# Order at the seams of token blocks in a fused attention and two-MLP kernel: low part ahead of the gate, weight split behind it, sum banks released singly

## The reference

```python
for t in range(S):
    y[:, :, t] = einsum('bhd,bhde->bhe', r[t], state + outer(u * k[t], v[t]))
    state = w[t][..., None] * state + outer(k[t], v[t])
h = x @ moe_w_in                      # first MLP, x from y
x = (h * clip(h + 3, 0, 6) / 6) @ moe_w_out
h = x @ moe2_w_in                     # second MLP
out = (h * sigmoid(h)) @ moe2_w_out
```

## Time and profile before

| | |
|---|---|
| time, median of 3 runs | 937.94 us (937.28 to 940.25) |
| the profiled execution | 939.23 us |
| its span, first to last instruction | 937.5 us |
| mean granted TensorE clock | 0.978 |
| PE busy | 905.1 us, 97% |
| DVE, ACT, POOL busy | 467.1, 320.2, 155.7 us |
| first seam of a step / stage seam | about 141 us / about 534 us |

### The profile page before, as it was taken

One profiled execution on the slowest core, in us unless ns is written; L12 is line 12 of the kernel. 1 busy time (PEld: TensorE's weight loads), 2 busy tenths in 40 slices (PEclk: granted clock), 3 DMA queues, 4 the chain that ended last, 5 costly groups with the idle time before them and its releaser, 6 DMA issues.

```text
span 937.5 us, 15408 instructions
## 1 busy us (share of the span) xinstructions
PE 905.1 (97%) x5876; PEld 776.2 (83%) x5876; DVE 467.1 (50%) x692; ACT 320.2 (34%) x537; POOL 155.7 (17%) x154
## 2 busy tenths in 40 slices
PE   5479999999999999999999999999999999999998
PEld 4468888887888888788888799998999989999897
DVE  5866746664674666467445542342333333333332
ACT  1343323333333333333344632333332332332332
POOL 6553413231341333134000000000000000000000
PEclk7679999999999999999999999999999999999999
DMA  8561221113123111311202200000000000000000
GB/s 250 174 184 38 74 76 45 55 55 99 46 63 82 37 55 55 99 59 51 100 7 96 68 1 1 35 0 0 34 0 0 34 0 0 34 0 0 34 1 34
DMA packets 13367, 48.54 MB, mean 52 GB/s; under 512 B 1568, under 2 KB 2208, under 8 KB 13344
## 3 DMA queue, kind: packets, MB, share of 16 engines
q1 hardware_dynamic: 13344, 48.23, 16.6%
HBM read 43.50 MB, written 4.72 MB: 51 GB/s over the span
## 4 chain that ended last, share of the span: by engine, by line
PE 92%; DVE 2%; DMA 2%; issue 1%; POOL 1%; ACT 1%; SPq 0%; POOLq 0%; ACTq 0%
PE bank L679 14%; PE bank L680 14%; PE bank L681 14%; PE bank L691 7%; PE bank L703 7%; PE bank L705 7%; PE bank L704 7%; PE bank L692 7%; PE bank L693 7%; PE bank L739 2%; PE bank L770 2%; PE bank L775 1%; DMA x<-u_row 1%; PE bank L752 1%; PE bank L727 1%
## 5 line engine op out<-in xcount | busy, mean ns | idle before, releaser
L679 PE MATMUL bank<-x_hi,w_hi 128*128 (+1 forms) x576 | 227.6, 395 | 1.7 <-DVE x_lo L590 1.7
L680 PE MATMUL bank<-x_lo,w_hi 128*128 (+1 forms) x576 | 227.0, 394 | 0.0
L681 PE MATMUL bank<-x_hi,w_lo 128*128 (+1 forms) x576 | 226.9, 394 | 0.0
L397 ACT CAST g_hi<-g 128x512 fp32r<-128x512 f32 x192 | 119.2, 621 | 284.2 <-PE bank L705 144.2
L517 DVE TENSOR_TENSOR g<-g,bank 128x512 f32<-128x512 f32 x96 | 65.9, 687 | 244.4 <-ACT g L391 244.4
L524 DVE TENSOR_TENSOR g_lo<-g,g_hi 128x512 fp32r<-128x512 f32 x192 | 147.7, 769 | 0.9 <-ACT g_hi L397 0.9
L703 PE MATMUL bank<-w_hi,g_hi 128*128 128x384 f32 x384 | 129.5, 337 | 0.0
L705 PE MATMUL bank<-w_hi,g_lo 128*128 128x384 f32 x384 | 129.5, 337 | 0.0
L704 PE MATMUL bank<-w_lo,g_hi 128*128 128x384 f32 x384 | 129.0, 336 | 0.0
L679 PEld LDWEIGHTS bank<-x_hi,w_hi 128*128 128x128 f32 x576 | 108.9, 189 | 24.3 <-DVE x_lo L590 2.1
L681 PEld LDWEIGHTS bank<-x_hi,w_lo 128*128 128x128 f32 x576 | 108.6, 189 | 23.4
(11 more groups left out here) (91 smaller groups left out, 807.9 us busy)
## 6 DMA issues: line engine op xcount, KB each, us to landing
unit_in<-rkv_tm SPq DMA_DIRECT2D x23, 576.0 KB, 5.9
unit_in<-rk_fm SPq DMA_DIRECT2D x23, 448.0 KB, 4.0
x<-w SPq DMA_DIRECT2D x8, 768.0 KB, 5.5
unit_in<-w SPq DMA_DIRECT2D x8, 768.0 KB, 4.3
unit_in<-w_fm SPq DMA_DIRECT2D x23, 226.2 KB, 4.6
out<-tmp SPq DMA_DIRECT2D x5, 768.0 KB, 3.3
out<-tmp SPq DMA_DIRECT2D x4, 192.0 KB, 2.0
x<-rkv_tm SPq DMA_DIRECT2D x1, 576.0 KB, 14.4
```

The lines of the kernel that those rows point to most:

```text
L397: nc.scalar.copy(g_hi[:, p, :], g[:, p, :]).then_inc(ghi_done, 1)
L679: nc.tensor.matmul(h_ps[j % 2][:, :], wh, xh, start=k == 0, stop=False)
L680: nc.tensor.matmul(h_ps[j % 2][:, :], wh, xl, start=False, stop=False)
L681: last = nc.tensor.matmul(h_ps[j % 2][:, :], wl, xh, start=False, stop=k == KT - 1)
```

## The change

It has three parts.

- **Low part first.** On DVE, at j = 16 of each pass of the first MLP, `glo` of tile 15 goes ahead of `gated` of the next step's tile 0. In the looped passes that is a condition on j, in the written-out sixth pass the code is in that order.
- **Weight chunk behind the gate.** At the stage seam, ACT splits weight chunk 6 (`whi`) after tile 0 of the second MLP and not before it; DVE's `wlo` of the same chunk moves behind `gated` of tile 0 and ahead of `gated` of tile 1.
- **Banks one by one.** ACT copies banks 0 and 2, DVE bank 1, and PE waits inside `sums1` of a step's first tile, before each bank's three matmuls, for that bank's copy only. The second MLP's first sums wait for all copies as before. The start value of `sums_a` and all its other thresholds go up by one.

```diff
@@ ScalarE
             def sums_out(c):
                 act.wait_ge(summed, FT * c + FT)
-                for m in range(2):
+                for m in range(0, KT, 2):
                     nc.scalar.copy(x2_step(c, m), acc[m][:, :]).then_inc(sums_a, 1)
...
             for j in range(2):
+                tile(FT * STEPS + j, j, ACT.Sigmoid)
                 if j == 0:
                     whi(CHUNKS + 6)
-                tile(FT * STEPS + j, j, ACT.Sigmoid)
             sums_out(c)
             whi(CHUNKS + 7)
@@ VectorE
             def sums_out(c):
                 dve.wait_ge(summed, FT * c + FT)
-                nc.vector.tensor_copy(x2_step(c, 2), acc[2][:, :]).then_inc(sums_v, 1)
+                nc.vector.tensor_copy(x2_step(c, 1), acc[1][:, :]).then_inc(sums_v, 1)

             with dve.Fori(0, STEPS - 1) as c:
                 for j in range(2, FT + 2):
+                    if j == FT:
+                        glo(FT * c + j - 1, j - 1)
                     gated(FT * c + j, j, 1.0, ALU.min)
-                    glo(FT * c + j - 1, j - 1)
+                    if j != FT:
+                        glo(FT * c + j - 1, j - 1)
                     attention(j, RUN, c + 1, B * (c + 1), c)
                 sums_out(c)
...
-            for j in range(FT, FT + 2):
-                if j == FT:
-                    wlo(CHUNKS + 6)
-                gated(FT * c + j, j, None, None)
-                glo(FT * c + j - 1, j - 1)
+            glo(FT * c + FT - 1, FT - 1)
+            gated(FT * c + FT, FT, None, None)
+            wlo(CHUNKS + 6)
+            gated(FT * c + FT + 1, FT + 1, None, None)
+            glo(FT * c + FT, FT)
             sums_out(c)
             wlo(CHUNKS + 7)
@@ TensorE
-            def sums1(n, j):
+            def sums1(n, j, c):
                 pe.wait_ge(glo_done, n + 1)
...
                 for m in range(KT):
+                    if j == 0:
+                        if m % 2 == 0:
+                            pe.wait_ge(sums_a, 2 * c + 1 + m // 2)
+                        else:
+                            pe.wait_ge(sums_v, c + 1)
...
                     hidden(FT * c + j, j, c + j // FT, 0)
-                    if j == 2:
-                        pe.wait_ge(sums_a, 2 * c + 1)
-                        pe.wait_ge(sums_v, c + 1)
```

More of the change, by code:

```diff
@@ L295, in _ @@
             with sp.Fori(0, STEPS - 1) as c:
-                sp.wait_ge(sums_a, 2 * (STEPS + c) + 3)
+                sp.wait_ge(sums_a, 2 * (STEPS + c) + 4)
                 sp.wait_ge(sums_v, STEPS + 2 * c + 3)
@@ L301, in _ @@
                 if m % 2 == 0:
-                    sp.wait_ge(sums_a, 2 * (STEPS + c) + 2 + m // 2)
+                    sp.wait_ge(sums_a, 2 * (STEPS + c) + 3 + m // 2)
                 else:
@@ L321, in _ @@
                                     base=0, pattern=[[1, C]], channel_multiplier=-1).then_inc(consts, 1)
-            nc.gpsimd.memset(half[:, :], 0.5).then_inc(sums_a, 1)
+            nc.gpsimd.memset(half[:, :], 0.5).then_inc(sums_a, 2)
             def decayed_keys(b, a, c):
@@ L446, in x2_hi @@
                 act.wait_ge(hidden_full, FT * (STEPS + c - 1))
-                act.wait_ge(sums_a, 2 * c + 3)
+                act.wait_ge(sums_a, 2 * c + 4)
                 act.wait_ge(sums_v, c + 2)
@@ L455, in _ @@
             act.wait_ge(consts, 3)
-            act.wait_ge(sums_a, 1)
+            act.wait_ge(sums_a, 2)
             nc.scalar.activation(half[:, :], half[:, :], ACT.Relu).then_inc(half_done, 1)
@@ L796, in _ @@
                     if j == FT:
-                        sums1(FT * c + j - 2, j - 2)
+                        sums1(FT * c + j - 2, j - 2, c)
                         pe.wait_ge(xlo_done, B * (c + 2))
                     hidden(FT * c + j, j, c + j // FT, 0)
-                    if j == 2:
-                        pe.wait_ge(sums_a, 2 * c + 1)
-                        pe.wait_ge(sums_v, c + 1)
                     if j != FT:
-                        sums1(FT * c + j - 2, j - 2)
+                        sums1(FT * c + j - 2, j - 2, c)
                     attention(j, RUN, B * (c + 1), c)
@@ L823, in _ @@
                     if j == 2:
-                        pe.wait_ge(sums_a, 2 * (STEPS + c) + 1)
+                        pe.wait_ge(sums_a, 2 * (STEPS + c) + 2)
                         pe.wait_ge(sums_v, STEPS + 2 * c + 1)
```

## The result

| | before | changed |
|---|---|---|
| median | 937.98 us (12 runs, 936.53 to 940.25) | 936.48 us (12 runs, 933.82 to 937.39) |
| profiled execution | 939.23 us | 933.82 us |
| its span | 937.5 us | 932.0 us |

The ratio of the times is 0.9979, with a 95% interval of 0.9969 to 0.9989: 2.0 us less, by the interval 1.0 to 2.9. Timed again later beside other kernels it was 0.9964 (0.995 to 0.9978). Forecast were 935.7 us, 2.2 us less. The two medians are 1.5 us apart; single runs of one kernel scatter by more than that, so the ratio is the better number.

What follows compares the result with a forecast made beforehand. PE was taken as the bound, so only gaps between its matmuls could be won: -2.03 - 0.48 + 0.3 = -2.2 us from the median 937.94 gives 935.7 us. The 8-in-10 range was 934.4 to 937.5 us.

Steps and rivals of the forecast that it cites:

- What bounds the kernel: Whole kernel: PE is busy 97% of the span, so only time between its matmuls can be won.
- Part one: Five looped seams: tile 15's low part ahead of the next product removes PE's loss before its sums, gaining 2.03 us.
- Nothing took the low part's place as the release: Looped seams: only PE itself is next in line; rival that another release holds the matmuls, 937.8 us, chance 0.05.
- Part three: First sums of a step in four looped passes: waiting per bank removes 0.12 us each, gaining 0.48 us.
- The bound of 0.96 the other way: First sums of a step: the two added register waits per pass could cost, making this part lose 0.96 us.
- Part two and the stage seam: Stage seam: 0.96 us gained before tile 15's sums is given back by a later wait; net cost 0.3 us.
- The new gap: Stage seam, before the second MLP's first sums: PE waits some 1.3 us for late bank copies.
- The sum: Whole kernel: -2.03 - 0.48 + 0.3 = -2.2 us, giving 935.7 us, within what counts as no change.
- Keeping the stage seam's gain: Stage seam: rival that bank copies come on time, -3.6 us in all, 934.3 us, chance 0.12.
- Register waits: Looped first sums: rival that added waits through a register cost time, -0.8 us in all, 937.1 us, chance 0.07.
- Drain at the table load: Stage seam: rival that a 1.38 us drain delays tile 0's gate, -0.8 us in all, 937.1 us, chance 0.04.
- Clock: Before the second MLP's sums: rival that about 1.2 us idle drops PE's clock, 938.2 us with 5 us slow, chance 0.05.

Runs made afterwards that it cites:

- the extra waits: Changed kernel plus 288 already satisfied waits ahead of first-MLP sum matmuls; 857.34 us from first looped transpose to last matmul, changed kernel 857.35.
- the chunk ahead of the gate: Changed kernel with weight chunk 6 back before tile 0's gate on ACT, and on DVE between tile 15's low part and tile 0's product; ratio to before 0.9972.
- chunks a tile earlier: Changed kernel with weight chunk 5 split at tile 14 and chunk 6 at tile 15 of the first MLP; ratio to before 0.9954.
- the added copy: Changed kernel plus an unused 128x1536 ACT copy ahead of chunk 6's cast; 858.73 us from first looped transpose to last matmul, changed kernel 857.35.
- the chunk alone: Kernel before with only weight chunk 6 moved behind tile 0's gate at the stage seam; ratio to before 0.9993.
- the banks alone: Kernel before with only the sum banks released one by one; ratio to before 0.9992.

## Why the prediction was right, step by step

- **What bounds the kernel.** PE's gaps, and nothing else moved. Right.
- **Part one.** Right in mechanism, 2.03 forecast and 2.28 measured when alone. The term was undersized because I counted two distances per gap. For some starts behind a gap the distance stays at 0.23 to 0.24 instead of 0.227 (16 steps of 0.229), which adds about 0.05 to each gap. Nothing took the low part's place as the release. Of the 2.03 itself, 0.36 at the second seam was not the order's own loss but a meeting with POOL (last section), there by chance.
- **Part three.** 0.48 forecast, 0.64 measured alone with an unlucky meeting in it. The bound of 0.96 the other way fell with the extra waits, which cost nothing.
- **Part two and the stage seam.** The working held nearly row by row. Tile 0's gate was to start 1.5 us earlier beside PE; it starts 2.32 us ahead of the last `hidden` matmul (524.98 and 527.30) where it was 0.95, so 1.37. The copies were to end 1.2 us after PE was ready; they end at 532.71, PE was ready at 531.61, so 1.1. The new gap is 1.60 from start to start, the loss with the one behind it 1.46; forecast were some 1.3. Over the stage seam the change lost 0.3, as forecast: 1.31 more before `sums2`, and some 1.0 less in front (0.96, and 0.04 in the starts behind that gap). So of part two's gain nothing was left, and the low part's new place alone would have sufficed to close the front: with the chunk ahead of the gate the front had no gap either.
- **The sum.** -2.2 forecast, -2.72 by the ruler, -2.0 by the times. The difference to the ruler is in parts one and three, whose terms were some 0.5 too small together. That the times come nearer to the forecast than the ruler does is chance: their interval, 1.0 to 2.9, holds both. The prediction took 0.3% for the least that can be told from no change. Twelve runs on each side told 0.21% from it.
- **Rivals.** Keeping the stage seam's gain: not in the changed kernel; chunks a tile earlier keep it whole, the chunk ahead of the gate keeps some 0.6 of it. Register waits: no cost. Drain at the table load: none, the activation at 524.98 starts 0.01 behind the load's end at 524.97. The page of the Trainium skill that speaks of it (ScalarE: Activation LUTs, "What ACT_TABLE_LOAD costs") is not borne out here for the drain, while its length of the load, 1.28 us, is what the row shows. Clock: it held at 1.2 us and, with the added copy, at 2.58 us.

## What to carry to other kernels

At a seam of a software pipeline, ask of each instruction in a strictly ordered queue whether it waits for something that the next one does not need: one such exchange gave four fifths of the whole gain here, by the ruler. Moving work from in front of a wait to behind it pays only if the chain behind has room; look at which chain is just in time there (here the bank copies) before the move, and try an earlier idle slot first. And when a change is worth 0.2%, measure between two marks of the trace inside the changed region, since the start of the kernel alone moved by 3 us from trace to trace.

## What the runs showed of the hardware that was not expected

- **Low part and POOL.** At three looped seams tile 15's low part met POOL's 128x384 product (L335): the second seam of before, the fourth with the chunk alone, the first with the banks alone. They ended at 222.91, 385.41 and 139.91, and the POOL operations at 222.36, 384.86 and 139.36: each time 0.55 us later, wherever the low part had started. So DVE did not slow down, but waited until POOL's instruction was over. It holds far from the seams too: in the twelve traces 251 low parts started while a POOL instruction was running, with more than 0.11 us of it left, and every one ended 0.54 to 0.56 us behind the end of a POOL instruction. Low parts that POOL met only after they had started kept their 0.68 us. That fits the lock that the Trainium skill describes (SBUF — State Buffer, "SBUF: two separate sides"). Which seam is hit depends on when a DMA lands, and it cost PE 0.4 to 0.8 us each time. It was one seam of five in each of the three traces with the old order in the loops. In the nine traces with part one no tile 15 low part of a looped seam meets POOL, a gain that I had booked as a part of one seam's loss.
- **An idle time of 2.58 us kept the clock, one of 2.70 did not.** The first stands in the kernel with the added copy, behind some 470 us at 2.4 GHz. The second stands early in the kernel with the chunk alone, where PE had reached the upper level only 6 us before the matmul at 61.11; the clock fell 0.8 us behind that matmul's start. At the same early place it fell in all twelve traces, in an idle time of 2.70 to 3.62 us or within 1 us behind it (3.07 in the kernel before). The two places differ in more than the idle time, so from which length on it falls is not shown.

```profile
61.11 0.47 PE L691 MATMUL bank<-g_hi,w_hi 128*128 128x512 f32 x1 [2.70 <-issue]
```

- **A satisfied wait is free.** 288 more waits ahead of matmuls moved the 458 us by less than 0.02.
